# A three-stage kernel (decayed attention, channel mix, token mix with MLP): own and state products as two steps, y of two halves copied by two engines, late weight parts moved

## The reference

```python
# attention: q, k, v, alpha are [4, 8, 768, 48]
for t in range(S):
    state = alpha[:, :, t, :, None] * state + einsum('bhd,bhe->bhde', k[:, :, t], v[:, :, t])
    y[:, :, t] = einsum('bhd,bhde->bhe', q[:, :, t], state)
x = y.transpose(0, 2, 1, 3).reshape(B, S, H * D)                  # [4, 768, 384]
# channel mix
xk = mu_k * x + (1 - mu_k) * x_prev;  xr = mu_r * x + (1 - mu_r) * x_prev
x = sigmoid(xr @ w_r) * (maximum(xk @ w_k, 0) ** 2 @ w_v)         # w_k [384, 1024]
# token mix and MLP
u = x + (x^T @ U @ V)^T                                           # U [768, 32], V [32, 768]
out = u + maximum(u @ w_ch1, 0) @ w_ch2                           # w_ch1 [384, 1536]
```

## Time and profile before

| what | value |
|---|---|
| median of 3 runs | 769.6 us (768.95 to 772.24) |
| the profiled execution's own time | 775.15 us |
| its span | 773.4 us |
| PE busy | 726.6 us, 94% |
| DVE busy | 426.2 us, 55% |
| ACT busy | 255.0 us, 33% |
| mean granted TensorE clock | 0.971 |

### The profile page before, as it was taken

How to read it: one execution, slowest core, us unless ns; L and a number is a source line. 1 busy time by engine, 2 the same in 40 slices (tenths; PEclk the granted TensorE clock), 3 DMA queues, 4 the chain that set the end, 5 groups by cost and what they waited for, 6 DMA issues and landing times.

```text
span 773.4 us, 22440 instructions
## 1 busy us (share of the span) xinstructions
PE 726.6 (94%) x10120; PEld 686.6 (89%) x10120; DVE 426.2 (55%) x748; ACT 255.0 (33%) x501; POOL 61.0 (8%) x123
## 2 busy tenths in 40 slices
PE   4668979899999999999999999999999999989998
PEld 4658969879999999979999999978999999969998
DVE  4777859753397517854387516955288425342222
ACT  1343555233333225233332324232342434321211
POOL 3401101000011000100011000100011000000000
PEclk9967989799999999999999999999999999999999
DMA  8565120000500033000500015000500000000000
GB/s 228 177 210 190 57 81 2 2 2 20 146 33 3 1 90 107 3 2 6 160 33 3 2 46 151 2 3 2 164 33 2 3 9 31 1 0 1 13 19 31
DMA packets 17647, 39.97 MB, mean 52 GB/s; under 512 B 2800, under 2 KB 8560, under 8 KB 17552
## 3 DMA queue, kind: packets, MB, share of 16 engines
q1 hardware_dynamic: 17456, 38.48, 16.8%
q10 hardware_dynamic: 96, 0.07, 0.0%
HBM read 32.64 MB, written 4.72 MB: 48 GB/s over the span
## 4 chain that ended last, share of the span: by engine, by line
PE 82%; DVE 7%; DMA 6%; ACT 2%; issue 2%; SPq 1%; ACTq 0%; DVEq 0%
PE acc L606 12%; PE acc L607 12%; PE acc L608 12%; PE hps L606 11%; PE hps L608 10%; PE hps L607 10%; PE aps L432 5%; PE hps L694 2%; DMA T<-in_alpha 2%; PE aps L562 2%; DMA raw_k<-in_w_k 1%; PE aps L581 1%; PE aps L443 1%; PE aps L539 1%; DVE QK L1047 1%
## 5 line engine op out<-in xcount | busy, mean ns | idle before, releaser
L1230 DVE SCALAR_TENSOR_TENSOR hid_l<-hps,hid_h 128x384 fp32r<-128x384 f32 x96 | 53.4, 557 | 202.6 <-ACT hid_h L931 202.5
L931 ACT ACTIVATE hid_h<-hps 128x384 fp32r<-128x384 f32 x96 | 47.2, 491 | 196.1 <-PE hps L608 186.8
L606 PE MATMUL hps<-in_h,w_h 128*128 128x384 f32 x288 | 98.6, 343 | 0.7 <-DVE in_l L1210 0.7
L608 PE MATMUL hps<-in_h,w_l 128*128 128x384 f32 x288 | 97.2, 337 | 0.1
L607 PE MATMUL hps<-in_l,w_h 128*128 128x384 f32 x288 | 97.2, 337 | 0.0
L607 PE MATMUL acc<-w_l,hid_h 128*128 128x384 f32 x288 | 96.7, 336 | 0.0
L606 PE MATMUL acc<-w_h,hid_h 128*128 128x384 f32 x288 | 96.6, 335 | 0.0
L608 PE MATMUL acc<-w_h,hid_l 128*128 128x384 f32 x288 | 96.3, 334 | 0.0
L1047 DVE TENSOR_TENSOR QK<-QK,T 112x768 f32<-112x768 f32 x80 | 77.0, 971 | 14.1 <-PE aps L432 12.7
L899 ACT ACTIVATE tmp<-hps 128x384 f32<-128x384 f32 x64 | 31.5, 492 | 158.2 <-PE hps L608 148.8
L1350 POOL TENSOR_TENSOR T<-T 112x384 f32<-112x384 f32 (+4 forms) x80 | 42.5, 534 | 487.1 <-DVE QK L1056 314.4
(11 more groups left out here) (123 smaller groups left out, 1262.0 us busy)
## 6 DMA issues: line engine op xcount, KB each, us to landing
QK<-in_k SPq DMA_DIRECT2D x16, 336.0 KB, 4.0
QK<-in_q SPq DMA_DIRECT2D x16, 336.0 KB, 4.5
T<-in_alpha SPq DMA_DIRECT2D x16, 336.0 KB, 7.3
vt<-in_v SPq DMA_DIRECT2D x16, 288.0 KB, 8.0
raw<-in_w_ch SPq DMA_DIRECT2D x6, 768.0 KB, 6.5
out<-x SPq DMA_DIRECT2D x24, 192.0 KB, 2.0
QK<-in_q_odd SPq DMA_DIRECT2D x16, 168.0 KB, 6.2
raw_k<-in_w_k SPq DMA_DIRECT2D x3, 512.0 KB, 4.9
```

The costliest lines, as they stand in the source:

```text
L606: pe.matmul(o, a[0], b[0], start=first, stop=False)
L608: return pe.matmul(o, a[1], b[0], start=False, stop=last)
L931: nc.scalar.activation(hid[0][:, f % 2, :], hps[f % 2][:, 0:HT], ACT.Relu).then_inc(s_rel2, 1)
L1230: nc.vector.scalar_tensor_tensor(out=hid[1][:, f % 2, :], in0=hps[f % 2][:, 0:HT], scalar=0.0, in1=hid[0][:, f % 2, :].bitcast(F32), op0=A ...
```

## The change

- `own_chunks` and `from_states` become two steps of attention. ACT's copy of y moves to the step of the state products. BESIDE2 and BESIDE3 get one more step (at f = 5 and at f = 7), so for halves 2 to 7 one hidden step lies between them; FIRST takes both at f = 7.
- y of half 1 is copied like y of half 0: e = 0 rows by ACT, e = 1 rows by DVE (`keep_odd`), with waits on s_xe added on SP, PE and ACT.
- In the opening ACT splits only the w_v pieces of the first load ahead of y; the others go to `later_weights`. SP issues the moves of half 0 ahead of the second w_v load.
- DVE no longer makes the last eight low parts beside the levels of half 2, but behind hidden steps 4 and 6 of that channel mix (LATE) and 2 and 3 of the first mlp (LATE2), in a new order, and PE waits for each one where it is first used (`low_ready`).

```diff
+        PIECES_W2 = (2, 3, 4, 5, 0, 1)
...
+        W2_LOW = [PIECES_W2.index(i) + NE + N1 for i in range(N1)]
+        LOW_ORDER = ([NR, NR + 1, NR + NK, NR + NK + 1] + [n for i in range(2, NK) for n in (NR + i, NR + NK + i)] +
+                     [NE + i for i in range(N1 - 2)] +
+                     [W2_LOW[0], W2_LOW[1], W2_LOW[2], NE + N1 - 2, NE + N1 - 1, W2_LOW[3], W2_LOW[4], W2_LOW[5]])
+        N_OPENING = 2 * NK + N1 - 2
+
+        def low_ready(eng, n):
+
+            eng.wait_ge(s_vlo, LOW_ORDER.index(n) + 1)
...
             def move_split(n):
-                if opens(n):
-                    sp.wait_ge(s_xe, 1)
-                else:
+                if n < 2:
+                    sp.wait_ge(s_xe, 2 * n + 1)
+                if n > 0:
                     sp.wait_ge(s_yc, n + 1)
...
-            load_part(vw, w_v, F1 // 2, F1 // 2, s_wv[1])
             for g in range(2):
                 sp.dma_start(odd(units[1].q_odd(), g), q_odd[0, 1, g]).then_inc(s_o2[g], 16)
+            sp.wait_ge(s_a2[1], 16)
+            move_split(0)
+            load_part(vw, w_v, F1 // 2, F1 // 2, s_wv[1])
             sp.dma_start(u_sb[:], U).then_inc(s_U, 16)
-            sp.wait_ge(s_a2[1], 16)
             sp.wait_ge(s_wv[1], 16)
-            move_split(0)
...
                         pe.wait_ge(s_x, n)
+                        if n == 2:
+                            pe.wait_ge(s_xe, 4)
...
                 own_chunks(n)
+                yield
                 from_states(n)
...
-                    if f == 0 and half == 0:
-                        pe.wait_ge(s_vlo, 2 * NK + 2 * N1)
+                    if s == 0 and f % 2 == 0:
+                        low_ready(pe, NE + f // 2)
...
+                        if s == 0 and f % 2 == 1:
+                            low_ready(pe, W2_LOW[f // 2])
...
-                keep_split(n, 0)
-                keep_split(n, 1).then_inc(s_yc, 1)
-                act.wait_ge(s_y, 3 * n + 3)
-                for e in range(2):
-                    keep_rest(n, e, False)
-                keep_rest(n, 0, True)
-                keep_rest(n, 1, True).then_inc(s_x, 1)
+                if n == 1:
+                    keep_split(n, 0).then_inc(s_yc, 1)
+                    act.wait_ge(s_y, 3 * n + 3)
+                    keep_rest(n, 0, False)
+                    keep_rest(n, 1, True).then_inc(s_x, 1)
+                else:
...
-                next_weights()
+                for n in range(NR + NK, NR + NK + NK // 2):
+                    act.wait_ge(s_wv[0], 16)
+                    high(n, *PIECES[n][:2])
...
+            def later_weights():
+
+                act.wait_ge(s_wv[1], 16)
+                for n in range(NR + NK + NK // 2, NE):
                     high(n, *PIECES[n][:2])
+                    yield
...
+            def keep_odd(n):
+
+                rows = slice(HS, HS + D)
+                dve.wait_ge(s_y, 3 * n + 2)
+                nc.vector.tensor_copy(unit(n).y_split()[rows, :], y_all[rows, 0:HT]).then_inc(s_xe, 1)
+                dve.wait_ge(s_y, 3 * n + 3)
+                nc.vector.tensor_copy(xT[rows, 0, 1:1 + HT], y_all[rows, HT:2 * HT])
+                nc.vector.tensor_copy(
+                    xT[0:D, 1:KT, 1:1 + HT],
+                    y_all[rows, 2 * HT:].rearrange("p (i t) -> p i t", t=HT)).then_inc(s_xe, 1)
...
+            def late_lows(at):
+
+                def late(f):
+                    for n in LOW_ORDER[N_OPENING:][at.get(f, slice(0, 0))]:
+                        low(n)
+                return late
...
-FIRST = [1, 1, 1, 1, 1, 1, 1, 3, 1, 0]
+FIRST = [1, 1, 1, 1, 1, 1, 1, 3, 2, 0]
-BESIDE2 = [0, 1, 1, 0, 1, 0, 0, 0, 0, 0, 0, 0]
+BESIDE2 = [0, 1, 1, 0, 1, 1, 0, 0, 0, 0, 0, 0]
-BESIDE3 = [0, 1, 1, 1, 1, 0, 1, 0, 0, 0, 0, 0]
-
-HIGHS = [0, 0, 0, 1, 1, 1, 1, 1, 1, 0, 0, 0, 0]
-LOWS = [0, 0, 0, 0, 1, 1, 1, 1, 2, 1, 0, 0, 1]
-LAST = [0, 1, 0, 2, 2, 2, 1, 0, 0, 0, 0, 0, 0]
+BESIDE3 = [0, 1, 1, 1, 1, 0, 1, 1, 0, 0, 0, 0]
+
+HIGHS = [0, 0, 0, 1, 1, 1, 1, 1, 1, 2, 0, 0, 0, 0]
+LOWS = [0, 0, 0, 0, 1, 1, 1, 1, 2, 1, 0, 0, 1, 0]
+LAST = [0, 1, 0, 2, 2, 1, 0, 0, 0, 0, 0, 0, 0, 0]
+
+LATE = {4: slice(0, 2), 6: slice(2, 4)}
+LATE2 = {2: slice(4, 6), 3: slice(6, 8)}
```

More of the change, by code:

```diff
@@ L255, in pieces @@
                 yield [w[:, :, 2 * i * P:2 * (i + 1) * P] for w in (w1w, *w1)]
-            for i in (2, 3, 4, 5, 0, 1):
+            for i in PIECES_W2:
                 yield [w[:, 2 * i:2 * i + 2, :] for w in (w2w, *w2)]
@@ L826, in attention @@
                 yield
+                yield
                 ge(act, s_prev, n)
                 act.wait_ge(s_y, 3 * n + 2)
-                keep_split(n, 0)
-                keep_split(n, 1).then_inc(s_yc, 1)
-                act.wait_ge(s_y, 3 * n + 3)
-                for e in range(2):
-                    keep_rest(n, e, False)
-                keep_rest(n, 0, True)
-                keep_rest(n, 1, True).then_inc(s_x, 1)
+                if n == 1:
[4 more added lines that the diff above has]
+                else:
+                    keep_split(n, 0)
+                    keep_split(n, 1).then_inc(s_yc, 1)
+                    act.wait_ge(s_y, 3 * n + 3)
+                    for e in range(2):
+                        keep_rest(n, e, False)
+                    keep_rest(n, 0, True)
+                    keep_rest(n, 1, True).then_inc(s_x, 1)
                 yield
@@ L867, in mix @@
                     act.wait_ge(s_split, 32 * KT * (s + 1))
-                    if opens(s):
-                        act.wait_ge(s_xe, 2)
+                    if s < 2:
+                        act.wait_ge(s_xe, 2 * (s + 1))
                     ge(act, s_prev, s)
@@ L977, in _ @@
             attend_first(levels(0))
-            steps = together(attention(1), later_weights(), HIGHS, N1)
+            steps = together(attention(1), later_weights(), HIGHS, NK // 2 + N1)
             step = stepper(steps)
@@ L1136, in attend_first @@
                 low(NR + 1)
[L1137 to L1144, removed]
+                keep_odd(0)
                 next(other)
@@ L1174, in mix, with channel_mix @@
                 low(KT - 1)
-            def channel_mix(b, half, step, plan, finish):
+            def channel_mix(b, half, step, plan, finish, late=lambda f: None):
                 s = 2 * b + half
@@ L1189, in channel_mix @@
                                             ALU.subtract).then_inc(s_tl, 1)
+                    late(f)
                 step(plan[1 + F1])
@@ L1223, in token_mix, with mlp @@
                     nc.vector.tensor_tensor(x1[:, c, :], acc[c % 3][:, 0:DM], x1[:, c, :], ALU.add).then_inc(s_u, 1)
-            def mlp(b, half, step, plan, next_mix=lambda: None, before_last=lambda: None):
+            def mlp(b, half, step, plan, next_mix=lambda: None, before_last=lambda: None, late=lambda f: None):
                 s = 2 * b + half
@@ L1253, in lows @@
             def lows():
[L1256 to L1260, removed]
+                for n in LOW_ORDER[4:N_OPENING]:
                     low(n)
                     yield
[L1264 to L1267, removed]
+            def late_lows(at):
[3 more added lines that the diff above has]
+                return late
             nc.vector.memset(xT[:, :, 0:1], 0.0).then_inc(s_fin, 1)
             dve.wait_ge(s_const, 6 + ML)
-            steps = together(attention(1), lows(), LOWS, 2 * NK - 4 + N1 - 2)
+            steps = together(attention(1), lows(), LOWS, N_OPENING - 4)
             step = stepper(steps)
@@ L1280, in _ @@
                 steps = attention(2 * b + 2)
-                if b == 0:
-                    steps = together(steps, last_lows(), LAST, N1 + 2)
                 step = stepper(steps)
-                channel_mix(b, 1, step, BESIDE1, lambda: gate(b, 1))
+                late = late_lows(LATE if b == 0 else {})
+                channel_mix(b, 1, step, BESIDE1, lambda: gate(b, 1), late)
                 token_mix(b, step, BESIDE_T)
-                mlp(b, 0, step, BESIDE2, lambda: mix(b + 1, 0, 0))
+                mlp(b, 0, step, BESIDE2, lambda: mix(b + 1, 0, 0), late=late_lows(LATE2 if b == 0 else {}))
                 run(steps)
```

11 lines of the change are left out of this document (5 added, 6 removed).

## The result

| | before | changed |
|---|---|---|
| median | 769.28 us (766.14 to 772.24, 4 runs) | 757.23 us (756.08 to 759.36, 4 runs) |
| the profiled execution's own time | 775.15 us | 757.66 us |
| its span | 773.4 us | 755.9 us |
| mean granted clock | 0.971 | 0.993 |

The ratio is 0.9847, with a 95% interval of 0.9802 to 0.9893: 12 us less, where 756.5 was predicted, with 752.5 to 762.5 as the range. Two more measurements on other chips gave 757.51 and 758.23 us, at ratios of 0.985 and 0.9857. The total fits, in part by luck. The terms fit less well: the largest was 4 us too big, another was 1.6 us too small, and some of the rest comes from a stretch of low clock that no term had.

A forecast was written before the change was run, and what follows sets the result against it. TensorE, busy 94% of the span, was taken as the bound, so only its waits, low clock and instruction count matter. Terms -2.8 - 0.4 - 7.9 - 2.2 = -13.3 us from 769.6 gave 756.3, said as 756.5; range 752.5 to 762.5.

The forecast's parts named there:

- A: Opening, y of half 0: ACT copies y without waiting for the second w_v load, so the mix starts sooner; -2.8 us.
- Rival 2: The opening gives nothing because its mix waits for something else, such as late-landing moves; 759.3 us, chance 0.10.
- B: Copies of y of half 1 shared by ACT and DVE: split copy, moves and mix come 0.4 us earlier; -0.4 us.
- C: Half 1's channel mix: moving low parts off busy DVE removes PE's wait and the low clock behind it; -7.9 us.
- Rival 1: The low-part term is worth half, -3.4 us, as the clock fall is absent or comes anyway; 761 us, chance 0.20.
- D: Halves 2 to 7: splitting own and state products shortens bursts of small products, ending most unexplained stalls; -2.2 us.
- rival 3: Stalls in own and state products stay because burst length is not their cause; 758.5 us, chance 0.15.
- The carry-over of the 5.5 us: The 13.3 us gain, worked out on the 775.15 us profiled execution, was subtracted unchanged from the 769.6 us median.
- Rival 4: Odd halves: late moves hold ACT at the mix, PE waits and its clock falls; +19.5 us, 775.8, chance 0.03.
- three signs that were to prove the forecast wrong: Low-part stage over 34 us, opening's mix starting past 50 us, or ACT's odd-half mix waiting for moves with PE idle.

The follow-up runs named there:

- undo_a: Changed kernel with the opening as before (ACT rounds all four w_v pieces ahead of y, second w_v load ahead of SP's moves): 761.26 us, ratio 0.9892.
- undo_c: Changed kernel with the last eight low parts on DVE beside the levels of half 2 again, PE's waits still one by one: 762.7 us, ratio 0.9902.
- undo_d: Changed kernel with own and state products next to each other again in halves 2 to 7: 762.45 us, ratio 0.9898.
- before_again: The unchanged kernel before, traced a second time: 770.39 us.
- shift: Kernel before with 128 empty instructions heading PE's queue; the compiled program did not keep them, so a third trace of the kernel before: 768.38 us.
- after_again: The changed kernel, run and traced once more without edits: 757.51 us.
- both_more: Changed kernel with ACT issuing three of half 1's six moves and one w_v low part taken out of the first mix: 756.38 us.

## Why the prediction was right, and where it was not

**A, -2.8: right at the mix**, in size (9.67 to 6.87) and step by step: ACT's copy at 42.58 (near 43 forecast), its mix at 47.43 (near 48), DVE's at 49.52 (near 49.3), with DVE's L1060 as what is late next. Rival 2 is out. The stage behind it takes 0.9 us longer by the medians, and runs of one kernel differ there by more (44.8 to 46.3), so what A leaves is between the 1.7 us that undo_a's trace shows at half 1's own products and the 3.2 us of its times.

**B, -0.4: 0.2 to 0.3 at the mix, nothing behind it.** The prediction took what the mix gains as gained by all that follows. At the first hidden product it is gone (18.1 us from the copy in both kernels), and the total can't show it.

**C, -7.9: the mechanism right, the term mis-sized.** The low parts are what DVE is late with, and the wait goes with them. But the term was the difference of two stages, 39.3 and 30.8 us, of one execution, and 3.9 us of it were a clock fall that neither repeat has. It is 3.8 us without one and 4.9 with the short one of undo_c. The failed step is the one that set's 9 us at 0.50 "after that wait" as its consequence in every run. Rival 1 is what happened to this term; its -3.4 was within half a us. The sign was there to read: the profiled execution took 775.15 us beside a median of 769.6.

**D, -2.2: too small, measured -3.8** (-3.7 by undo_d's times). The last column of the table shows 5.1, but 1.1 to 1.2 of it is the clock stretch near 687 us. The stalls go, so rival 3 is out. Three errors lie in the term: a stall was counted at its idle time, and costs 1.0 to 1.3 us; a fourth one, behind half 7, was not seen; and 0.2 us was charged for each change from small to large products, which with the 0.18 us wait that goes would leave nothing, while the halves without a stall gain 0.1 us. The working had the length of the burst as the cause, and not the place in the instruction queue: that is why halves 4 and 6, with bursts as long, had no stall.

**The sum.** Forecast -13.3; the stages make -2.8 - 0.2 - 3.8 - 5.1 + 0.9 + 0.5 = -10.5; measured 12 us, and 11.6 and 11.8 in the two further measurements. C was 4 too much, D 1.6 too little, the clock stretch near 687 us gave 1.2 that no term had, and 1.4 were given back behind the mixes. That these nearly cancel is luck. The times of undo_a, undo_c and undo_d put A, C and D at 3.2, 4.0 and 3.7, 10.9 together. The carry-over of the 5.5 us between profiled execution and median was the weak point that the prediction named: the term subtracted from the median clock time that the median didn't hold. **Rival 4** is a true mechanism over 2 us away from its point. Of the three signs that were to prove the forecast wrong, none came: the stage of C takes 31.75 us, the mix starts at 49.52, and ACT's mix in odd halves waits for nothing.

Open are about 1.5 us between the sum of stages and the times, which the different starts and clock stretches of the executions don't let one place, and what decides whether the clock falls behind a wait.

## What to carry to other kernels

Put work that only fills an engine (roundings, low parts) where the engine that sets the time is at least a step away, and look one by one at what stands between two operations of a chain. Price a wait by its own length, and the clock behind it as a separate term with a chance of its own, and take two or three traces before you count the clock: the first may be the unusual one. Where products are small and follow each other by the hundred, break the burst with large ones; a stall without releaser that comes back at the same instruction is a matter of place, not of data, and the times of the instruction packets tell whether it is a wait for instructions.

## What the hardware showed that I had not expected

- The same wait of 2.1 us ahead of the same work was followed by 9 us at clock 0.50 (before), by 3.4 us at 0.50 (undo_c) and by none (before_again, shift). In the opening the stretches at low clock of one program also differ: before has 3.4 us from 40, 13.7 from 47 and 6.8 from 67, after only 3.4 from 66, after_again 6.8 from 62.
- Stalls of 0.4 to 1.0 us (0.7 to 3.1 in the opening) at the same instruction in each execution, at place 197 or 198 of 256, behind long bursts of small products. Each ends 1.2 to 1.6 us after an instruction packet of 16,384 bytes has landed, and no 256 PE instructions passed in under 2.86 us in any of the 14 traces.
- Moves of 24 KB landed up to 3.1 us after the last of them was issued (both_more, 97.75 to 100.90).
